# Twelve of eighteen token tiles routed inside the first expert layer's blocks

## The reference

```python
x = attention(q, k, v)                      # 2304 tokens x 512, linear attention with decay
# first layer: d_ff = 1536, the same weights for all tokens
xn = x / sqrt(mean(x * x) + 1e-6) * rms_g
x = (silu(xn @ w_gate) * (xn @ w_val)) @ w_out
# second layer: 8 experts, d_ff = 1024
logits = x @ w_gate2                        # 2304 x 8
e_idx = argmax(logits, axis=1)
gate_w = softmax(logits)[token, e_idx]
eom = sigmoid(x @ w_output_gate)            # 2304 x 8
for e in range(8):
    mask = e_idx == e
    out[mask] = gate_w[mask] * eom[mask, e] * (relu(x[mask] @ w1[e]) @ w2[e])
```

## Time and profile before

| | |
|---|---|
| median of 3 timed runs | 831.54 us (831.5 to 831.65) |
| the profiled execution | 824.0 us, its span 822.3 us |
| TensorE busy | 784.7 us, 95% of the span |
| VectorE, ScalarE, GpSimd busy | 458.2, 445.5, 437.8 us |
| attention | 0 to about 85 us |
| three blocks of the first layer | about 85 to 506.5 us |
| routing stage | 506.5 to 543.3 us |
| second layer | 543.3 to 822 us |

### The profile page before, as it was taken

One profiled execution on the slowest core, in us unless ns is written; L12 is line 12 of the kernel. 1 busy time (PEld: TensorE's weight loads), 2 busy tenths in 40 slices (PEclk: granted clock), 3 DMA queues, 4 the chain that ended last, 5 costly groups with the idle time before them and its releaser, 6 DMA issues.

```text
span 822.3 us, 15149 instructions
## 1 busy us (share of the span) xinstructions
PE 784.7 (95%) x5053; PEld 699.7 (85%) x5053; DVE 458.2 (56%) x812; ACT 445.5 (54%) x880; POOL 437.8 (53%) x437
## 2 busy tenths in 40 slices
PE   6998899999999999999999999788999999999995
PEld 6887799987899998889999888567888888888884
DVE  3489677776647667436666323544455455545452
ACT  3566566556655555665556456423444545545543
POOL 2579887897848788666786231373122121321221
PEclk9999999999999999999999999889999999999998
DMA  9984032223212243211141123156455455564552
GB/s 317 317 282 149 26 104 77 77 65 95 63 36 78 59 148 112 68 52 39 66 146 47 39 65 119 37 104 156 132 161 184 159 173 161 161 199 145 162 181 91
DMA packets 48364, 99.68 MB, mean 121 GB/s; under 512 B 7489, under 2 KB 8643, under 8 KB 48294
## 3 DMA queue, kind: packets, MB, share of 16 engines
q1 hardware_dynamic: 42934, 87.40, 34.4%
q0 software_dynamic: 4944, 10.96, 4.6%
q10 hardware_dynamic: 432, 0.63, 0.2%
HBM read 89.50 MB, written 10.40 MB: 121 GB/s over the span
## 4 chain that ended last, share of the span: by engine, by line
PE 79%; POOL 9%; issue 4%; DMA 3%; DVE 2%; ACT 1%; POOLq 0%; SPq 0%; ACTq 0%; DVEq 0%
PE banks L1499 10%; PE banks L1501 9%; PE banks L1500 9%; PE banks L1561 6%; PE banks L1562 6%; PE banks L1563 6%; PE banks L1704 5%; PE banks L1703 5%; PE banks L1705 5%; PE banks L1483 4%; PE banks L1484 4%; PE banks L1485 4%; POOL slot_table L610 2%; POOL AL L519 2%; DMA qt<-q_t 2%
## 5 line engine op out<-in xcount | busy, mean ns | idle before, releaser
L1499 PE MATMUL banks<-BH,AH 128*128 128x384 f32 x504 | 170.1, 337 | 4.2 <-DVE g L833 2.4
L1501 PE MATMUL banks<-BH,AL 128*128 128x384 f32 x504 | 169.2, 336 | 0.0
L1500 PE MATMUL banks<-BL,AH 128*128 128x384 f32 x504 | 169.0, 335 | 0.0
L1499 PEld LDWEIGHTS banks<-BH,AH 128*128 128x128 f32 x504 | 95.2, 189 | 6.7 <-DVE g L833 3.1
L519 POOL TENSOR_TENSOR AL<-s_ab,AH 128x1024 fp32r<-128x1024 f32 x36 | 88.6, 2461 | 20.6 <-ACT AH L1139 20.6
L1500 PEld LDWEIGHTS banks<-BL,AH 128*128 128x128 f32 x504 | 95.2, 189 | 0.3
L1501 PEld LDWEIGHTS banks<-BH,AL 128*128 128x128 f32 x504 | 95.1, 189 | 0.0
L533 POOL TENSOR_TENSOR dL<-wraw,dH 128x256 fp32r<-128x256 f32 x72 | 58.0, 826 | 55.9 <-ACT dH L1155 55.6
L1561 PE MATMUL banks<-dH,hidH 128*128 128x512 f32 x216 | 85.0, 393 | 1.9 <-DVE hidL L870 1.0
L1563 PE MATMUL banks<-dH,hidL 128*128 128x512 f32 x216 | 84.3, 390 | 0.0
L1562 PE MATMUL banks<-dL,hidH 128*128 128x512 f32 x216 | 84.2, 390 | 0.0
(11 more groups left out here) (191 smaller groups left out, 1671.7 us busy)
## 6 DMA issues: line engine op xcount, KB each, us to landing
wraw<-w_moe SPq DMA_DIRECT2D x168, 256.0 KB, 3.1
wraw<-w_moe SPq DMA_DIRECT2D x36, 512.0 KB, 3.6
vr<-v_rows SPq DMA_DIRECT2D x15, 320.0 KB, 4.5
qt<-q_t SPq DMA_DIRECT2D x16, 288.0 KB, 5.2
y_rows<-y_sb SPq DMA_DIRECT2D x6, 768.0 KB, 6.0
kt<-k_t SPq DMA_DIRECT2D x15, 288.0 KB, 4.1
kr<-k_rows SPq DMA_DIRECT2D x16, 256.0 KB, 3.3
mask<-c_mask SPq DMA_DIRECT2D x4, 160.0 KB, 5.3
```

The costliest lines, as they stand in the source:

```text
L1499: mm(to, wh, bh, start=first and k == 0, stop=False, skip_group_check=True)
L1500: mm(to, wh, bl, start=False, stop=False, skip_group_check=True)
L1501: i = mm(to, wl, bh, start=False, stop=k == 1, skip_group_check=True)
```

## The change

The tiles of the first two blocks (`SOON` = 12 tiles) are routed while later blocks are computed; the last six tiles stay in the routing stage, in two groups.

- In blocks 1 and 2, steps f = 1 to 6, one tile of the block before is handled per step (`tile_at`). TensorE: four transposes ahead of m4(n), four logits matmuls behind m4(n), one transpose back behind m6 of the next step, all in bank 4 (`SPOT`). ScalarE: `copy_yt` behind `high_b22`, `copy_lg` ahead of `copy_z`, `copy_lgs` behind `high_a`. The copies go into unused parts of `late`.
- In block 2's down half, the twelve tiles' experts, counts, ranks, slots, gates (Exp), match operands, and their scatters, by VectorE (`soon`), TensorE (`counts_soon`), ScalarE (`exps(0)`) and GpSimd (`gates(0)`, `scatter_records`). The bank for the counts is one that held the copy of odd half-steps' hidden values, which in this block are read from `hid` instead.
- SyncE loads the routing constants when the last m4 is done, ahead of the down weights; the first weights of the second layer are issued ahead of the last store of y.
- In `hidden(n)`, for n = 0 alone, the sums of step 2 go behind `g1` and both `hv`.
- The routing stage works on six tiles; TensorE adds the twelve tiles' match ahead of the counts.

```diff
+SOON = TILES - 2 * TPH
+THIRD = TILES // 3
...
+        SIG, VAL, COPY, SPOT = (2, 3), 5, (7, 1), 4
+        COUNT = 1
...
+        def tile_at(n):
+            blk, f = n // F1, n % F1
+            return 2 * TPH * (blk - 1) + f - 1 if blk > 0 and 1 <= f <= 2 * TPH else None
...
@@ SyncE @@
+                if blk == BLOCKS - 1:
+                    sp.wait_ge(s_m4, N1)
+                    for to, what in ((row_no, c_rowno), (col_no, c_colno), (id_parts, c_idparts), (offsets, c_offsets), (pad_id, c_pad_id)):
+                        sp.dma_start(to[:], what).then_inc(s_lconst, 16)
+                    sp.dma_start(route_c[:], c_route).then_inc(s_const, 16)
+                    sp.dma_start(plan_c[:], c_plan).then_inc(s_const, 16)
+                    sp.dma_start(rec[:], c_ids).then_inc(s_const, 16)
...
@@ GpSimd @@
-                    if blk + 1 < BLOCKS and f in DOWN_B:
+                    if not last and f in DOWN_B:
                         low_b(blk + 1, DOWN_B[f])
+                    if last and f == 0:
+                        route_consts()
+                    if last and f == 5:
+                        gates(0)
+                        pool.wait_ge(s_pad, 32)
+                    if last and 6 <= f < 10:
+                        scatter_records(range(2 * (f - 6), 2 * (f - 6) + 2))
+            scatter_records(range(8, SOON))
+            gates(1)
-            scatter_records(range(EARLY))
+            scatter_records(range(SOON, SOON + EARLY))
...
@@ VectorE, hidden(n) @@
-                sums_two(n + 2)
+                if n > 0:
+                    sums_two(n + 2)
...
+                if n == 0:
+                    sums_two(2)
...
+            def soon(f, half):
+                both = lgs.rearrange("p (t e) -> p t e", t=SOON)
+                if (f, half) == (1, 1):
+                    dve.wait_ge(s_lgs, SOON)
+                    dve.wait_ge(s_const, 16 * (NCONST + 3))
+                    dve.wait_ge(s_m4, N1)
+                    choose(0, both)
+                if (f, half) == (2, 1):
+                    own_gate(0, both)
...
+                if (f, half) == (4, 0):
+                    n = EXPERTS * SOON
+                    ranks(0, banks[:, COUNT, n:2 * n], banks[:, COUNT, 0:n])
+                if (f, half) == (5, 0):
+                    slot_rows(0)
+                if (f, half) == (5, 1):
+                    slot_columns(0)
+                if (f, half) in ((6, 0), (6, 1)):
+                    slot_match(half)
...
@@ ScalarE @@
+            def copy_yt(i):
+                act.wait_ge(s_tA, i + 1)
+                wait(act, s_lA, i)
...
+                S.activation(y_t1, banks[:, SPOT, :].rearrange("p (k i) -> p k i", k=KD), ACT.Copy).then_inc(s_ytA, 1)
...
+                if blk == BLOCKS - 1 and f == 4:
+                    exps(0)
...
@@ TensorE @@
+            def tile_t(i):
+                pe.wait_ge(s_y, max(i + 1, i // (2 * TPH) * 2 * TPH + TPH + 2))
+                wait(pe, s_lgs, i)
...
+                for k in range(KD):
+                    j = nc.tensor.transpose(banks[:, SPOT, k * P:(k + 1) * P], y_sb[:, i, k * P:(k + 1) * P], ident[:])
+                j.then_inc(s_tA, 1)
+            def tile_l(i):
+                pe.wait_ge(s_ytA, i + 1)
+                for k in range(KD):
+                    j = mm(banks[0:2 * EXPERTS, SPOT, 0:P], wroute[:, k, :], y_t1[:, k, :], start=k == 0, stop=k == KD - 1)
+                j.then_inc(s_lA, 1)
...
+                    if tile_at(n) is not None:
+                        tile_t(tile_at(n))
                     m4(n)
+                    if tile_at(n) is not None:
+                        tile_l(tile_at(n))
...
+                    if n == n0 + 3 and blk == BLOCKS - 1:
+                        counts_soon()
```

More of the change, by code:

```diff
@@ new lines, in own_gate, with ranks @@
+            def own_gate(ph, both):
+                t = slice(*PHASES[ph])
+                dve.wait_ge(s_onehot, ph + 1)
+                link(V.tensor_tensor(work[ph][:], both[:, :, EXPERTS:2 * EXPERTS].rearrange(E_T), onehotB[ph][:], ALU.mult))
+                V.tensor_reduce(col[:, 2, t], work[ph][:].rearrange(T_E), AX.X, ALU.add).then_inc(s_ogate, 1)
+            def ranks(ph, counts, starts):
+                t = slice(*PHASES[ph])
+                dve.wait_ge(s_cnt, ph + 1)
+                dve.wait_ge(s_ogate, ph + 1)
+                link(V.tensor_tensor_scan(incl[ph][:].rearrange(flat), route_part(ph, 1).rearrange(flat), counts,
+                                          0.0, ALU.mult, ALU.add))
+                link(V.tensor_tensor(work[ph][:], incl[ph][:], starts.rearrange("p (e t) -> p e t", e=EXPERTS), ALU.add))
+                link(V.tensor_tensor(work[ph][:], work[ph][:], onehotB[ph][:], ALU.mult))
+                V.tensor_reduce(col[:, 5, t], work[ph][:].rearrange(T_E), AX.X, ALU.add).then_inc(s_rank, 1)
@@ new lines, in _ @@
+                V.tensor_copy(y_t[:, g, :, P:2 * P],
+                              banks[:, BT[g][1], :].rearrange("p (k i) -> p k i", k=KD)).then_inc(s_ytv, 1)
+            dve.wait_ge(s_lgtr, 2)
+            both = banks[:, 5, 0:2 * TPH * 2 * EXPERTS].rearrange("p (t e) -> p t e", t=2 * TPH)
+            choose(1, both)
+            own_gate(1, both)
+            n = EXPERTS * (TILES - SOON)
+            ranks(1, banks[:, 7, 0:n], banks[:, 6, 0:n])
+            slot_rows(1)
+            slot_columns(1)
@@ L977, in _ @@
+            slot_match(2)
             dve.wait_ge(s_idsum, 1)
@@ L1576, in _ @@
                     m6(n)
+                    if tile_at(n - 1) is not None:
+                        tile_lt(tile_at(n - 1))
                     if last:
@@ L1610, in logits_t @@
                 i.then_inc(s_lgtr, 1)
-            pe.wait_ge(s_const, 16 * NCONST)
             pe.wait_ge(s_y, TILES - TPH)
+            pe.wait_ge(s_hidL, 2 * N1)
+            pe.wait_ge(s_rank, 1)
             tiles_t(0)
-            for g in range(GRPS):
+            for g in range(2):
                 if g == 0:
```

314 lines of the change are left out of this document (180 added, 134 removed).

## The result

| | median | runs |
|---|---|---|
| kernel before, beside the changed one | 831.52 us | 830.87 to 831.65, 4 runs |
| changed kernel | 849.48 us | 849.1 to 850.24, 4 runs |

The ratio is 1.0216, with a 95% interval of 1.0200 to 1.0231: slower by 18.0 us. The forecast was 848.8 us. The profiled execution of the changed kernel took 849.16 us (span 847.5), the one of before 824.0 (span 822.3). So the two timed medians are 18.0 us apart and the two traces 25.2. The prediction is near the first number, but its sum was made against the second trace, and there it is 7.9 us short. That the forecast came so near is in part luck, as the point by point part shows. Where these 7.9 us are, and what made up for them, is the larger part of what follows.

What follows compares the result with a forecast made beforehand. TensorE was taken to bound the kernel. Against the profiled 824.0 us: +34.3 (tiles) + 0.9 (last down half) - 10.7 (routing) - 5.7 (first iteration) - 1.5 (block 0) gives 841.3; plus 7.5, 848.8 us; range 839.5 to 859.

Steps and rivals of the forecast that it cites:

- What bounds the kernel: Whole kernel: TensorE, busy 784.7 of 822.3 us; any microsecond added to its row in a block lengthens the kernel equally.
- A tile: Blocks 1 and 2: 2.86 us each (transposes 0.49, logits 0.98, transpose back 0.09, stop 1.2, restart 0.1), twelve make 34.3 us.
- rival 2: Blocks 1 and 2: one strip's logits are cheap but the stop stays; 2.21 us a tile, 841.0 us; chance 15%.
- Clock in the blocks: TensorE's granted clock was to stay at 1.00 over block 1's first half despite the twelve stops.
- rival 3: Blocks 1 and 2: the clock falls with the twelve stops, up to 17.4 us more, 866.2 us; chance 13%.
- Last down half: Block 2's down half: counts 0.4 us and late dL on GpSimd 0.5 us, together 0.9 us more; ScalarE's and VectorE's additions hidden.
- rival 4: Last down half: GpSimd falls behind, each dL from the eighth on late by 0.7 us; 851.8 us; chance 8%.
- Start of block 0: Block 0's first steps: the stop before m7 goes, the same wait comes one step on; gain 1.5 us (0.6 to 2.1).
- Routing stage: Six groups become two, counts about a microsecond late; the first gather leaves 10.7 us earlier (9.5 to 11.5).
- First iteration: Second layer: three scatters left, so records come sooner; wait of 4.0 and slower clock of 1.6 us go, gain 5.7.
- From the trace to the median: Timed median of the kernel before is 7.5 us above its profiled run; carried over, 841.3 becomes 848.8 us.

Runs made afterwards that it cites:

- the kernel with three tiles at once: Changed kernel with ScalarE's tile copy ahead of the high part waiting for m4, and three tiles' logits issued together in three column strips: 822.42 us, ratio 0.9908.
- the copy first: Changed kernel with one edit: on ScalarE the copy of the turned tile stands ahead of the high part that waits for m4; 835.36 us, ratio 1.0051.
- The sums alone: Kernel before with only VectorE's reordering in block 0's first step, the weight sums behind g1 and both hv: 830.5 us, ratio 0.9992.

## Why the two traces differ by more than the medians

The changed kernel's trace took as long as its timed runs (849.16 and 849.48). The trace of before was 7.5 us quicker than its own (on which chip either was taken isn't on record). So the kernel before was profiled again:

> The kernel before, unchanged, for a second profile. Its first profiled execution took 824.0 us where the timed ones took 831.5; the changed kernel's profiled execution took 849.16 where its timed ones took 849.5. Theory A: there is a stretch of some 7.5 us that comes in most executions of the kernel before and was missing in the profiled one; then this profile should show about 831 us and differ from the first in one stretch. Theory B: the profiler's execution is simply shorter for this kernel; then this one shows about 824 again.

Measured: 832.36 us, span 830.7, like the timed runs. Its waits between 540 and 580 us (engine, output, line, released by, total, times, longest) show what the first trace has nowhere:

```profile
ACT h2H L1367 <- remote: 16.4, 1, 16.4
...
PE banks L1703 <- DVE h2L L1037: 14.4, 1, 14.4
```

And its timeline. ScalarE has made the last `xgH` of the first tokens at 542.62. Its next instruction is the first inside the second layer's loop, L1367. The product that this needs is done by 546.34, yet ScalarE starts it at 559.50, and TensorE stands still for 14.41 us, while GpSimd sends out scatters until 556.85:

```profile
542.62 0.45 ACT L1333 ACTIVATE xgH<-banks 128x336 fp32r<-128x336 f32 x1 [0.37 <-PE banks L1664]
...
555.88 0.97 POOL L610 DMA_INDIRECT slot_table<-rec,slot_i  x1 [0.30 <-issue]
559.50 0.45 ACT L1367 ACTIVATE h2H<-banks 128x336 fp32r<-128x336 f32 x1 [16.43 <-remote]
...
560.74 0.76 PE L1703 MATMUL banks<-wH,h2H 128*112 128x512 f32 x1 [14.41 <-DVE h2L L1037]
```

In the first trace of before the same instruction starts at 546.92, 3.30 us behind ScalarE's last, as soon as the product is there. The stop costs less than its length: the 3.89 us wait for the second gathers and 1.6 us of slow clock are hidden in it, and 14.4 - 5.5 = 8.9 us are left, near the 8.4 us by which the spans differ.

Is it the fifteen scatters? They were left out (the records they should write stay empty, and the output with them):

```
-            scatter_records(range(EARLY, TILES))
...
-            pool.wait_ge(s_scat, 16 * TILES)
+            pool.wait_ge(s_scat, 16 * EARLY)
```

> The kernel before with fifteen of its eighteen scatters of records left out (the three ahead of the first gathers stay), so its second-layer gathers read unfilled records and the output differs. Question: the second profile of the kernel before (832.36 us) has a stop that the first (824.0 us) has not: ScalarE stands idle from 543.07 to 559.50 at the entry of the second layer's loop, while GpSimd issues scatters until 556.85, and TensorE waits 14.41 us for it. Theory A: ScalarE is held while the scatters go out, so without them the stop goes, and with it the two costs after it: 830.5 - 14.4 + what follows late in any case. In the first profile, without the stop, the kernel took 824.0 and lost 5.6 to the late second gathers, so A gives 824.0 - 5.6 = 818.4, 816.5 to 820.5. Theory B: the stop belongs to the loop's entry itself and the scatters only run beside it: the stop stays, 14 us long, and the second gathers were hidden in it anyway: 829 to 831.

Measured: 815.78 us (813.37 to 816.52, 4 runs), but the kernel before took 822.28 on this chip (819.22 to 824.72, 16 runs), not 830.5. Ratio 0.9903 (0.9875 to 0.9931). The stop was not there to be removed, since the kernel before doesn't have it on this chip, and so the run doesn't choose between A and B. It prices something else: without the late records the second gathers are early, the first iteration takes 29.0 us instead of 33.4, the one behind it loses no 1.6 us to a slower clock, together 6.0 of the 6.5 us measured. The prediction had 5.7 us for it.

Is it ScalarE's read of the number of blocks? The read was moved from behind the tokens' copies to ahead of them, and run on two chips:

```
+            act.wait_ge(s_plan, 1)
+            nb = act.value_load(nblocks[0:1, 0:1], min_val=1, max_val=MAXB)
             heads_x(0, 0, FIRST_X, KD)
-            act.wait_ge(s_plan, 1)
-            nb = act.value_load(nblocks[0:1, 0:1], min_val=1, max_val=MAXB)
```

> The kernel before, where ScalarE reads the number of blocks into its register ahead of the copies of the first tokens (about 537) and not behind them (543). Theory A1: what holds ScalarE is this read, beside the scatters that start at 538: read earlier, the stop shrinks or goes, and the time falls towards the 824.0 of the first profile, 823 to 826. Theory A2: what holds ScalarE is the entry of the loop behind it: the stop stays at 543 to 559, 829 to 832. Theory A3: the read is held wherever it stands: the copies of the first tokens come late too, 831 to 836.

Measured: 822.15 us (818.21 to 824.72, 10 runs) where before took 822.28, ratio 1.0001 (0.9982 to 1.0020); the trace has no stop. The numbers look like A1, but without a stop in the kernel before they say nothing. So the same kernel once more, on a chip where the kernel before takes 830.68:

> The kernel before with ScalarE's read of the number of blocks ahead of the copies of the first tokens. Where the kernel before took 822.3 this changed nothing, since there was no stop to move. On a chip where the kernel before takes 830: without a stop, about 822 to 826, it is the read beside the scatters that holds ScalarE; with the stop still at the loop's entry, 830 to 833, it isn't. On a chip where the kernel before takes 822 it says nothing and takes 822.

Measured: 830.69 us, span 829.0. The tokens' copies come in time, and the stop stands where it stood, at the loop's first instruction:

```profile
542.26 1.48 ACT L1333 ACTIVATE xgH<-banks 128x336 fp32r<-128x336 f32 x4 [12.94 <-issue]
557.93 0.45 ACT L1367 ACTIVATE h2H<-banks 128x336 fp32r<-128x336 f32 x1 [14.19 <-remote]
```

A1 and A3 fall: the read's place doesn't make the stop. The stop is 2.1 to 2.2 us shorter than the 16.4 and 16.3 us of the two other traces that have it; whether the read has a part of that size isn't shown by this one execution. What the runs show is where it stands: at the entry of the loop on ScalarE.

Does the changed kernel have it anywhere? It ran again beside before on that chip:

> The changed kernel, unchanged, beside the kernel before on one more chip. The kernel before took 831.5 and 830.5 us on two chips and 822.3 on a third; its trace of 832.36 us has the 16.4 us stop of ScalarE at the loop's entry, its trace of 824.0 us and one of 821.88 us of nearly the same kernel have none. Theory S (the difference of the chips is this stop, and the changed kernel, whose scatters are nearly all out by then, has it nowhere): the changed kernel takes 849.5 (847 to 851) on any chip, so the change costs 18 to 19 us where before has the stop and 25 to 28 where it hasn't. Theory C (one chip is 1% quicker in everything): the difference stays at 18 to 19 us, so 840 to 842 where before takes 822.

Measured: 847.51 us (845.97 to 850.34, 4 runs) against 830.68 (828.54 to 832.31, 7 runs), ratio 1.0199 (1.0169 to 1.0229). Before had the stop here; the changed kernel went into the loop with only the 3.49 us that the product takes:

```profile
576.71 0.45 ACT L1495 ACTIVATE h2H<-banks 128x336 fp32r<-128x336 f32 x1 [3.49 <-PE banks L1613]
```

The changed kernel itself never ran beside a kernel before of 822, so this run doesn't exclude theory C. The traces do. Once the loop is running, an iteration of the kernel before, or of one close to it, takes 32.67 us on the two chips with the stop (traces of 832.36 and 830.69 us) and 32.66 on the one without (821.88 and 816.43 us), where 1% would be 0.33 us. And the kernel with three tiles at once and the two made from it in the next section take 387.3 us from the first up matmul to the last up product, on all three chips. So the chips don't differ by 1% in everything, and three of the kernel before or one close to it (832.36, 830.39, 830.69 us) have a ScalarE stop of 16.4, 16.3 and 14.2 us at the loop's entry, three others (824.0, 821.88 and, without scatters, 816.43) have none, and in all six the second layer starts between 540.8 and 543.5 us. On the two chips with the stop all 24 timed runs of the kernel before took 828.5 to 833.3 us, on the one without all 16 took 819.2 to 824.7, so by the times the stop comes with the chip, or with what was loaded there, and not now and then on one. None of the eight traces of the changed kernel and of those derived from it has it, on any chip, the two chips with the stop among them.

What makes the stop is open. Leaving out the scatters on a chip with the stop would choose between theories A and B, and that wasn't run. By its length it looks tied to the fifteen scatters, but in the trace of 830.69 us it ended at 557.93 while the last scatter was going out (557.16 to 558.13), and in that of 832.36 us 2.6 us behind it. The Trainium skill, "Runtime: NRT & Kernel Launch", Instruction fetch mechanics, says that a taken branch whose target isn't loaded makes the engine wait for a fetch; no run here shows a fetch of ScalarE's code (in the trace of 832.36 us the two instruction queues have no packet between 540 and 563 us), so it isn't shown to be this.

## The first gathers land late

In the changed kernel the first gather is issued 19.0 us after the last down half's end (543.36 to 562.38), in before 28.45. 9.45 of the 10.7 us came, but the stage gained only 6.4. Its timeline shows the rest: the last gather goes out at 565.40, SyncE's loads of 256 KB for the second layer at 565.90, 566.47 and 567.11, and the last tokens land at 572.15, 6.75 us after their issue, where in before it was 4.2 (537.56 to 541.79), with 2.4 us between the gather and the first load (the expectations below count from the end of the gather's own instruction, 1 us later):

```profile
562.38 1.03 POOL L668 DMA_INDIRECT xg<-y_rows,first_ids  x1 [0.30 <-issue]
...
565.40 0.98 POOL L668 DMA_INDIRECT xg<-y_rows,first_ids  x1 [0.30 <-issue]
...
568.67 1.01 PE L1834 MATMUL banks<-ident,xg 112*128 112x112 f32 x4 [3.19 <-DMA xg<-y_rows,first_ids]
...
572.15 1.01 PE L1834 MATMUL banks<-ident,xg 112*128 112x112 f32 x4 [1.21 <-DMA xg<-y_rows,first_ids]
```

Two kernels test whether the loads do it, both on the kernel with three tiles at once. The one holds the loads back until the last gather has landed:

```
             nb = sp.value_load(nblocks[0:1, 0:1], min_val=1, max_val=MAXB)
+            sp.wait_ge(s_first[GROUPS - 1], 16)
```

> The same kernel with three scatters ahead as it was, but SyncE waits for the last of the first gathers to land before it issues the second layer's third to fifth weight loads. Theory G: the last gather lands some 2 us sooner (about 542.4 instead of 544.45), the loads leave at 542.5 instead of 538.80 and are still ahead of their use: 820.4 (819.3 to 821.5). Theory N: the gathers land as late as before, the loads come 5.6 us later, and ScalarE waits for them in the first iteration: 823 to 826.

Measured: 818.66 us (818.01 to 820.3, 7 runs), with the kernel before at 822.28, ratio 0.9960 (0.9940 to 0.9980); a little below theory G's range, and far from theory N's. The last gather is issued at 537.68 and all twelve transposes lie between 539.98 and 542.4; without the hold (issue 538.29) TensorE waited again for the last tokens until 544.45. First the kernel with the hold, then the one without:

```profile
539.98 2.45 PE L1848 MATMUL banks<-ident,xg 112*128 112x112 f32 x12 [1.91 <-DMA xg<-y_rows,first_ids]
```

```profile
540.76 1.83 PE L1847 MATMUL banks<-ident,xg 112*128 112x112 f32 x8 [5.08 <-DMA xg<-y_rows,first_ids]
544.45 1.01 PE L1847 MATMUL banks<-ident,xg 112*128 112x112 f32 x4 [1.86 <-DMA xg<-y_rows,first_ids]
```

The other lets the gathers go sooner. The row numbers are there at 532.5, but two more scatters stood ahead:

```
-EARLY = 3
+EARLY = 1
```

> The kernel with three tiles' logits at once and the copy first (822.4 us), with one scatter ahead of the first gathers instead of three. In its trace the row numbers are written at 532.37 to 532.53, the three scatters take GpSimd from 531.02 to 535.14, and the first gather goes at 535.44. With one scatter it goes at 532.87, 2.57 us earlier. Theory G (the weight loads at 538.80 to 540.33 slow the gathers down that are issued up to 539.26): the gathers now lead the loads by 2.6 us more, and the last lands about 3.2 us after its issue, as in the kernel before, and not 5.2: together 4.5 us, 817.9 (816.5 to 819.5). Theory N (the landing isn't slowed by the loads): 2.6 us only, 819.8.

Measured: 815.89 us (814.04 to 817.39, 4 runs), 0.992 (0.9896 to 0.9944) of a kernel before without the stop (822.28). That is 6.5 us below the median of the kernel with three scatters ahead, on another chip, and by the spans of the two traces 7.8 (812.4 and 820.2), where I had expected 4.5. The tokens land one behind the other, the transposes take 1.63 us and the second layer starts at 540.65 instead of 546.14:

```profile
538.07 1.63 PE L1847 MATMUL banks<-ident,xg 112*128 112x112 f32 x12
540.65 0.42 PE L1619 MATMUL banks<-xgH,wH 128*128 x1 [0.95 <-DVE xgL L1115]
```

That is 5.5 us. The other 2.3 us are the first iteration's: TensorE stood 7 us for the tokens in the slower kernel and entered the second layer at the lower level of its clock, and in the quicker one it didn't. The stages from 540.7 to 549 us, first with three scatters ahead, then with one:

```profile
540.70:549.00 8.30, 5.70 (x22) 4.85 (x23) 1.75 (x4) 1.48 (x4) 3.12 (x4) 0.50 0.44 123
```

```profile
540.70:549.00 8.30, 8.30 (x48) 7.68 (x49) 4.49 (x9) 3.70 (x8) 3.34 (x5) 1.00 0.52 130
```

Both kernels agree with theory G, that the loads slow the gathers, though both gained more than its range says (the hold has a span of 817.0). The fourteen traces fall into two groups. Where the first load goes out 0.5 us behind the last gather (five traces), the last tokens' transposes start 5.6 to 6.75 us after that gather's issue. Where it goes out 2.4 us behind or later (nine traces), they start 3.45 to 4.2 us after it.

## Run again on other chips: what beats before

The kernel with three tiles at once ran again on a chip where the kernel before has its stop, and the kernel with one scatter ahead got the sums of the second step moved too (`if n > 1` and `if n <= 1` in place of `n > 0` and `n == 0`).

> The kernel with three tiles' logits at once and the copy first, as before with three scatters ahead of the first gathers. It took 822.4 where the kernel before took 830.5, and its trace has no ScalarE stop. Theory S: 822.4 (821 to 824.5) on any chip; then against a kernel before of 822 it gains nothing, and the kernel with one scatter ahead is 6 to 7 us below it. Theory C: 1% below before on any chip.

Measured: 822.93 us (821.87 to 824.05, 4 runs), ratio 0.9899 (0.9882 to 0.9916), as on the first chip.

> Three tiles' logits at once, the copy first, one scatter ahead of the first gathers (815.9 us), and now the product g and the two hv ahead of the weight sums for the second step of block 0 too, not for the first alone. In the trace the stop at m7 of that step is 0.99 us, behind VectorE's sums, which wait for GpSimd. Theory W (the wait moves one step on each time): that stop goes, a shorter one may stand at the third step: 1 us less at the most, 814.5 to 816.5; the ScalarE stop of 0.91 us at m3 stays. Theory X: the sums, later now, come late for their own reader, and the third step stops longer than the second did: 816.5 to 818.

Measured: 818.14 us (817.03 to 819.02, 4 runs), ratio 0.9849 (0.9833 to 0.9865) of a kernel before with the stop. Its trace has no wait at m7 of the second step any more, and two in its place, one for ScalarE in that step and the old one for g a step on:

```profile
106.20 0.45 PE L1635 MATMUL banks<-BH,AH 128*128 128x384 f32 x1 [0.34 <-ACT p_m L1292]
110.64 0.44 PE L1635 MATMUL banks<-BH,AH 128*128 128x384 f32 x1 [1.04 <-DVE g L889]
```

So the wait moves on and nothing is gained; in its one trace the up and down halves up to the last up matmul even take 0.6 us longer than in the kernel without the edit, which speaks for theory X. The 2.2 us by which its median is slower can't be put down to the edit as a whole: the two ran on different chips, and the traces have 2.2 us of difference in the routing stage, where TensorE ran at the lower level of its clock, the counts waited 2.27 us instead of 0.69 and the first gather left 17.2 us after the stage's start instead of 14.9.

Of all kernels here the one with one scatter ahead is the quickest: 6.4 us under the kernel before at its best (822.28), and by the medians on different chips 14.6 us under it with its stop (830.5). What of this is the change's idea is not shown. With the logits packed and the copy first it is level with a kernel before of 822.28. The rest came from gathers that go ahead of two scatters, and the kernel before could have that edit without any tile in its blocks: there too the first gather stands behind three scatters. That kernel wasn't run. Against a kernel before with the stop, most of the gain is the stop, and why it is gone is open.

## The prediction, point by point

- **What bounds the kernel.** Right. Every microsecond that a tile takes on TensorE's row went into the time: 12 x 3.10 = 37.2, less 1.85 at the start of block 0 and with a start that was 0.3 us later in this execution, is the 35.6 us up to the last up matmul.
- **A tile.** 2.86 forecast, 3.10 measured. The logits: 0.98, as forecast, so rival 2 falls. The stop: 1.33 - 0.17 = 1.16 us from one issue to the next where 1.2 was forecast. The transposes: 0.36 us and 0.09 at the return to m4. Mis-sized are the transpose back and the returns: behind each of the three insertions the first of the block's matmuls takes 0.27 us to the next one instead of 0.17 (290.36 to 290.63), and the lone transpose back costs 0.43 - 0.17 = 0.26 with it 0.38, where a third of a group's 0.28 had been counted as 0.09. That is most of the 2.9 us that the twelve tiles cost more.
- **Clock in the blocks.** 1.00 through all of them: twelve stops of 1.2 us did not bring it down, and rival 3 falls.
- **Last down half.** 1.3 for 0.9; TensorE idles 0.4 us in it. GpSimd did not fall further behind step by step, as rival 4 has it: its dL delayed TensorE's weight loads twice, by 0.7 us in all.
- **Start of block 0.** 1.85 for 1.5 in the trace, with the wait one step on, at 102.91, as forecast, though it is 1.01 us and not about 2; the 0.95 us for ScalarE at 98.48 was not. The sums alone brought between 1.9 us less and 0.5 more in timed runs, and in the traces 0.3 to 1.9, by what the clock does behind the old stop.
- **Routing stage.** This step failed: -6.4 instead of -10.7. The first gather came 9.45 us sooner, and 1.3 us were lost because VectorE waited 2.27 us for the counts, where about one had been allowed. Ahead of the counts TensorE's list has a product that only keeps it busy (L1805). With TensorE at the lower level it took 2.06 us; in the first trace of the kernel with three tiles at once, at the upper level, 1.10 us, with a wait of 0.51 for the counts (more below):

```profile
552.72 2.06 PE L1805 MATMUL banks<-y_sb,ones 128*128 128x512 f32 x2
555.60 0.26 DVE L984 TENSOR_TENSOR_SCAN incl<-route_c,banks 128x48 f32<-128x48 f32 x1 [2.27 <-PE banks L1820]
```

  Then 2.5 us were lost in landing, because the gathers had moved to within 0.5 us of the weight loads: I had moved an event 10 us ahead and not asked what it would meet. The last 0.5 us are the transposes at the lower level.
- **First iteration.** -5.6 for -5.7, with no wait for the second gathers, as forecast; leaving out the scatters gave 6.0 on its own.
- **From the trace to the median.** This step failed as well, in the other direction. I carried the 7.5 us between the profiled and the timed runs of before over to the changed kernel. By the traces they were a stop that only the kernel before has (the timed runs themselves have no trace). The sum was 7.9 us too low and the carried 7.5 us should have been nothing: 0.4 us are left of both, and 0.3 are the changed kernel's own median above its trace. The forecast of 848.8 is right by two errors that cancel; that is luck. The direction and nine tenths of the price of the tiles are right by their own steps.

**To carry to other kernels.** When a step is moved forward, look at what its DMAs meet at the new place, and at which engine's order stands between it and its reader. When a profiled execution is quicker or slower than the timed ones by more than their spread, as here by 7.5 us, look for the stretch that makes it before adding a sum to it. Work taken out of a packed group can cost the group's time for each piece: here one tile's logits took 0.98 us and three tiles' 0.99.

## What the runs showed of the hardware

- **ScalarE at the entry of a loop.** A stop of 14 to 16 us in three of the six traces of the kernel before and its near kin, and in none of the eight of the kernels with tiles in the blocks. The kernel before took 831.5, 830.5 and 830.7 us in three sets of runs and 822.3 in a fourth, on another chip. Its cause is open.
- **TensorE's clock before the counts.** In the routing stage two executions with the same program did the same work, 1.6 us of 3.3 to 3.6, and then one stayed at 2.4 GHz and one fell to 1.2. The stages of the kernel with three tiles at once, its first trace:

```profile
523.00:526.30 3.30, 1.61 (x31) 1.33 (x31) 0.00 (x0) 1.68 (x7) 0.00 (x0) 1.00 0.73 147
526.30:529.00 2.70, 2.70 (x24) 1.62 (x22) 1.82 (x9) 1.06 (x4) 1.29 (x7) 1.00 0.00 0
```

and its second:

```profile
523.00:526.60 3.60, 1.61 (x31) 1.33 (x31) 0.54 (x1) 1.99 (x7) 0.00 (x0) 1.00 0.78 161
526.60:530.70 4.10, 4.10 (x23) 2.49 (x22) 1.52 (x8) 2.01 (x5) 2.06 (x10) 0.51 0.00 0
```

  The second needs 4.1 us for what takes the first 2.7, and the counts wait 2.24 us instead of 0.51. The changed kernel did as the second, in both its traces. The first gather left 17.1 us after the stage's start in the one and 18.9 in the other: a forecast of this stage is no better than these 1.7 us.
- **A return costs a tenth.** Between the block's matmuls and the fp32 products put between them the first matmul after the change of kind takes 0.10 us more to the next, 0.27 for 0.17, in the changed kernel, in the one with the copy first (0.28) and in the one with three tiles at once (0.28).
- **Gathers beside loads.** The indirect gathers of the first tokens took 1.4 us and more longer when SyncE's 256 KB loads went out 0.5 us behind them (5.6 to 6.75 us to their last use, against 3.45 to 4.2).
